# Attention pairs written out instead of looped, with weight loads and the handover to the feed-forward part in another order

## What is computed

```python
scores = scale * np.matmul(q, k.transpose(0, 1, 3, 2))      # 4 x 8 x 576 x 576
scores = np.where(block_i >= block_j, scores, -1e9)
attn = softmax(scores); x = attn @ v                         # -> 2304 x 512
gate = sigmoid(x @ w_gate); x = (gate * (x @ w_val)) @ w_out # d_ff 1536
e = argmax(x @ moe2_w_gate); out = p_e * relu(x @ w1[e]) @ w2[e]
```

## Time and profile before

| | us |
|---|---|
| median of 3 runs | 920.15 (918.3 to 922.79) |
| the profiled execution, its own time | 919.3 |
| its span, first to last instruction | 917.6 |
| attention part, up to the first feed-forward product | 196.35 |
| from there to the end of the span | 721.2 |

### The profile page before, as it was taken

One profiled execution on the slowest core, in us unless ns is written; L12 is line 12 of the kernel. 1 busy time (PEld: TensorE's weight loads), 2 busy tenths in 40 slices (PEclk: granted clock), 3 DMA queues, 4 the chain that ended last, 5 costly groups with the idle time before them and its releaser, 6 DMA issues.

```text
span 917.6 us, 15686 instructions
## 1 busy us (share of the span) xinstructions
PE 883.9 (96%) x5202; PEld 731.4 (80%) x5203; DVE 465.3 (51%) x1084; ACT 299.8 (33%) x694; POOL 215.9 (24%) x233
## 2 busy tenths in 40 slices
PE   7989998999999999999999999999999999999995
PEld 3545454569999999999999999999878888888884
DVE  5767775752124335334433543575484536483252
ACT  4545554543222113112112111223333424362141
POOL 4133335322112111211211211122112222221221
PEclk9999999999999999999999999999999999999998
DMA  4544455532412002002000100024336446474110
GB/s 138 166 125 162 152 162 169 165 109 77 147 46 69 1 1 69 1 1 70 1 1 20 51 1 1 35 67 143 124 132 224 138 131 194 132 242 135 46 46 29
DMA packets 48111, 85.37 MB, mean 93 GB/s; under 512 B 9255, under 2 KB 21543, under 8 KB 47920
## 3 DMA queue, kind: packets, MB, share of 16 engines
q1 hardware_dynamic: 42288, 69.34, 23.3%
q0 software_dynamic: 3360, 10.50, 3.7%
q10 hardware_dynamic: 2400, 4.72, 1.4%
HBM read 70.28 MB, written 14.78 MB: 93 GB/s over the span
## 4 chain that ended last, share of the span: by engine, by line
PE 84%; DMA 5%; DVE 4%; issue 4%; ACT 1%; POOLq 0%; SPq 0%; POOL 0%; DVEq 0%; ACTq 0%
PE bank L1467 23%; PE bank L1469 23%; PE bank L1468 23%; PE bank L1439 4%; PE bank L1400 4%; PE bank L1412 4%; DMA rinv_scratch<-rinv 2%; PE bank L1618 2%; DMA rwide<-rinv_scratch 1%; PE bank L1581 1%; DVE nmax L1020 1%; ACT prob L828 1%; DMA yg<-y_scratch,gcol 1%; DMA out<-orow,scol 1%; DVE xo L999 0%
## 5 line engine op out<-in xcount | busy, mean ns | idle before, releaser
L1467 PE MATMUL bank<-xh,w1h 128*128 128x384 f32 x576 | 193.9, 337 | 0.0
L1469 PE MATMUL bank<-xh,w1l 128*128 128x384 f32 x576 | 193.2, 335 | 0.0
L1468 PE MATMUL bank<-xl,w1h 128*128 128x384 f32 x576 | 192.9, 335 | 0.0
L727 POOL TENSOR_TENSOR hl<-hraw,hh 128x384 fp32r<-128x384 f32 x72 | 83.2, 1156 | 369.1 <-ACT hh L857 369.1
L1209 DVE TENSOR_TENSOR hraw<-hraw,bank 128x384 f32<-128x384 f32 x72 | 39.9, 554 | 238.1 <-ACT hraw L902 237.8
L902 ACT ACTIVATE hraw<-bank 128x384 f32<-128x384 f32 x72 | 35.4, 492 | 236.9 <-PE bank L1469 236.9
L1467 PEld LDWEIGHTS bank<-xh,w1h 128*128 128x128 f32 x576 | 108.2, 188 | 2.4
L1468 PEld LDWEIGHTS bank<-xl,w1h 128*128 128x128 f32 x576 | 108.2, 188 | 2.2
L1469 PEld LDWEIGHTS bank<-xh,w1l 128*128 128x128 f32 x576 | 108.1, 188 | 0.0
L828 ACT ACTIVATE prob<-bank,nmax 128x576 f32<-128x576 f32 (+2 forms) x144 | 75.9, 528 | 88.3 <-DVE nmax L1020 85.4
L1469 PE MATMUL bank<-woh,hl 128*128 128x512 f32 x216 | 85.4, 395 | 0.0
(11 more groups left out here) (201 smaller groups left out, 1348.1 us busy)
## 6 DMA issues: line engine op xcount, KB each, us to landing
stage<-in_we SPq DMA_DIRECT2D x56, 512.0 KB, 4.2
w1raw<-in_w SPq DMA_DIRECT2D x8, 768.0 KB, 4.5
kt<-in_kT SPq DMA_DIRECT2D x16, 288.0 KB, 3.3
qt<-in_qT SPq DMA_DIRECT2D x16, 288.0 KB, 3.8
rwide<-rinv_scratch SPq DMA_DIRECT2D x32, 144.0 KB, 2.9
xt_scratch<-xo SPq DMA_DIRECT2D x16, 288.0 KB, 2.2
xraw<-xt_scratch SPq DMA_DIRECT2D x6, 768.0 KB, 4.5
y_scratch<-yrow ACTq DMA_DIRECT2D x6, 768.0 KB, 5.1
```

Of the source, the lines that this page charges most:

```text
L727: pool.tensor_tensor(hl[:, f % 2, :], hraw[:, f % 2, :], hh[:, f % 2, :].bitcast(F32), ALU.subtract).then_inc(h_low, 1)
L1467: pe.matmul(out_, wh, ah, start=first, stop=False, skip_group_check=True)
L1468: pe.matmul(out_, wh, al, start=False, stop=False, skip_group_check=True)
L1469: return pe.matmul(out_, wl, ah, start=False, stop=last, skip_group_check=True)
```

## The change

On all engines pairs 4 to 11 are written out like the others, so no loop, and no number that is worked out in a register, is left in the attention part. `apart` is no longer called on TensorE, nor in the attention part by SyncE and GpSimd.

- **Weights.** `w1raw` number k is issued in SyncE's turn of pair 2k + 2 instead of 2k + 1, right behind `rwide` and ahead of V; number 7 in the turn of pair 15. `wr_sb` moves from behind pair 3 to just ahead of `xraw` and pair 12.
- **Start.** ScalarE issues the first Q; SyncE issues the first K, then K and Q of pair 1, then V of both.
- **ScalarE.** The copy of block 4 is made after the exponential of block 8 instead of block 7.
- **Handover.** `up(0, 0)` goes ahead of the turns of blocks 5 and 6, `up(0, 1)` is cut in two halves around the turns of blocks 7 and 8, and `pv` comes last. The first two pieces of `w_out` are loaded early, into tiles that are free then (`yT` and the last row block of `yrow`). ScalarE's last copy and VectorE's last `o_out` move behind the first sigmoid and the second gate product.

The diff, without the lines that repeat the written-out loop on the other engines:

```diff
@@ -357,7 +357,7 @@
         OUT_V = {0: (1, 5), 1: (1, 7), 3: (0, 0), 4: (0, 1), 5: (0, 2), 6: (0, 3)}
-        OUT_A = {0: (1, 6), 2: (1, 8), 3: (0, 0), 7: (0, 4)}
+        OUT_A = {0: (1, 6), 2: (1, 8), 3: (0, 0), 8: (0, 4)}
         W1_STEP = 4
@@ -379,6 +379,11 @@
+        def wo_raw(f):
+            if f < 2:
+                return [yT[:].rearrange("p c n -> p (c n)"), yrow[:, GM - 1, :]][f]
+            return woraw[:, f % 2, :]
@@ -508,55 +513,64 @@
                 sp.wait_ge(rinv_done, g + 1)
-                apart(sp)
                 sp.dma_start(rinv_dram[par].rearrange("h q i -> (h q) i"), rinv[:, par, 0:NB]).then_inc(rinv_stored, 16)
...
                 sp.wait_ge(rinv_stored, 16 * (g + 1))
-                apart(sp)
-                if not (isinstance(g, int) and g == 0):
+                if g:
                     sp.wait_ge(xo_done, g)
-                    apart(sp)
                 for h in range(2):
...
+            def w1_load(k):
+                if k:
+                    sp.wait_ge(w1_low, k)
+                sp.dma_start(w1raw[:], w1[k:k + 1].rearrange("a p f -> p (a f)")).then_inc(w1_loaded, 16)
...
                     sp.wait_ge(scores_done, NB * (g - 1))
+                    qk_load(g, p)
+                    rinv_store(g - 2, p % 2)
+                    rwide_load(g - 2, p % 2)
+                    if p % 2 == 0:
+                        w1_load(g // 2 - 1)
+                    elif g == NPAIR - 1:
+                        w1_load(2 * C - 1)
+                    sp.wait_ge(pv_done, g - 1)
+                    v_load(g, p)
+                if p >= 2:
+                    o_store(b, p - 2)
+                elif b:
+                    o_store(b - 1, p + 2)
+            def qk_load(g, p):
                 sp.dma_start(kt[p % 2][:], qkv_at(kT, g)).then_inc(qk_loaded[p % 2], 16)
                 sp.dma_start(qt[p % 2][:], qkv_at(qT, g)).then_inc(qk_loaded[p % 2], 16)
-                if not early:
-                    rinv_store(g - 2, p % 2)
-                    rwide_load(g - 2, p % 2)
-                    sp.wait_ge(pv_done, g - 1)
+            def v_load(g, p):
                 sp.dma_start(vt[p % 2][:, 0:KT_N - 1, :],
...
                              ).then_inc(v_loaded[p % 2], 16)
-                if p >= 2:
-                    o_store(b, p - 2)
-                elif not (isinstance(b, int) and b == 0):
-                    o_store(b - 1, p + 2)
-                if p % 2 == 1:
-                    k = 2 * b + p // 2
-                    if not (isinstance(k, int) and k == 0):
-                        sp.wait_ge(w1_low, k)
-                    sp.dma_start(w1raw[:], w1[bass.ds(k, 1)].rearrange("a p f -> p (a f)")).then_inc(w1_loaded, 16)
-            for p in range(PPB):
-                pair(0, p)
-            sp.dma_start(wr_sb[:], wr.rearrange("(c p) e -> p c e", p=P)).then_inc(wr_loaded, 16)
-            with sp.Fori(1, BATCH - 1) as b:
+            sp.dma_start(kt[0][:], qkv_at(kT, 0)).then_inc(qk_loaded[0], 16)
+            qk_load(1, 1)
+            v_load(0, 0)
+            v_load(1, 1)
+            for b in range(BATCH - 1):
                 for p in range(PPB):
                     pair(b, p)
+            sp.dma_start(wr_sb[:], wr.rearrange("(c p) e -> p c e", p=P)).then_inc(wr_loaded, 16)
@@ -572,18 +586,22 @@
+            def wo_load(k):
+                sp.dma_start(wo_raw(k), w_out[k * P:(k + 1) * P, :]).then_inc(wo_loaded[k % 2], 16)
+            wo_load(0)
+            wo_load(1)
             o_store(BATCH - 1, PPB - 2)
...
             sp.wait_ge(pv_done, NPAIR)
-            sp.wait_ge(scores_done, NB * NPAIR)
-            for k in range(FC):
-                if k == 2:
+            for k in range(2, FC):
+                if k == 4:
                     o_store(BATCH - 1, PPB - 1)
-                if k >= 2:
-                    sp.wait_ge(wo_high, k - 1)
-                    sp.wait_ge(wo_low, k - 1)
-                sp.dma_start(woraw[:, k % 2, :], w_out[k * P:(k + 1) * P, :]).then_inc(wo_loaded[k % 2], 16)
+                sp.wait_ge(wo_high, k - 1)
+                sp.wait_ge(wo_low, k - 1)
+                wo_load(k)
                 if k == FC // 2:
@@ -700,7 +718,6 @@
                     pool.wait_ge(qk_loaded[p % 2], 16 * (g - p % 2) + 32)
-                    apart(pool)
                     pool.tensor_scalar(kt[p % 2][:], kt[p % 2][:], SCALE, None, ALU.mult).then_inc(kt_scaled, 1)
@@ -806,6 +821,8 @@
         def _(act):
+            act.dma_start(qt[0][:], qkv_at(qT, 0)).then_inc(qk_loaded[0], 16)
@@ -832,9 +849,7 @@
-            for p in range(PPB):
-                pair(0, p)
-            with act.Fori(1, BATCH - 1) as b:
+            for b in range(BATCH - 1):
                 for p in range(PPB):
@@ -846,7 +861,6 @@
             after_unit(NPAIR - 1, 1, 6)
-            after_unit(NPAIR - 1, 1, 8)
             act.wait_ge(scores_done, NB * NPAIR)
@@ -900,9 +914,11 @@
                     act.activation(hraw[:, f % 2, :], gv_psum(f)[0], ACT.Sigmoid).then_inc(sig_done, 1)
+                    if first and f == 0:
+                        after_unit(NPAIR - 1, 1, 8)
                     if first:
                         act.wait_ge(wo_loaded[f % 2], 16 * (f // 2 + 1))
-                        act.copy(woh[:, f, :], woraw[:, f % 2, :]).then_inc(wo_high, 1)
+                        act.copy(woh[:, f, :], wo_raw(f)).then_inc(wo_high, 1)
                     if not first and f == route_steps(G)[2]:
@@ -1207,11 +1221,11 @@
                     dve.tensor_tensor(hraw[:, f % 2, :], hraw[:, f % 2, :], val_ps, ALU.mult).then_inc(hraw_done, 1)
-                    if first and f == 0:
+                    if first and f == 1:
                         o_out(NPAIR - 1, 1)
                         dve.wait_ge(wo_high, f + 1)
-                        dve.tensor_tensor(wol[:, f, :], woraw[:, f % 2, :], woh[:, f, :].bitcast(F32),
+                        dve.tensor_tensor(wol[:, f, :], wo_raw(f), woh[:, f, :].bitcast(F32),
                                           ALU.subtract).then_inc(wo_low, 1)
@@ -1389,7 +1403,6 @@
                     pe.wait_ge(exp_done, NB * (g - 1) + 7 + 2 * k)
-                apart(pe)
                 for j in SUPER[k]:
@@ -1468,7 +1478,7 @@
-            def up(G, f):
+            def up(G, f, ms=(0, 1)):
@@ -1476,14 +1486,15 @@
                     pe.wait_ge(hraw_done, n - 1)
-                for m in range(2):
+                for m in ms:
                     for c in range(C):
...
                                      xh[:, c, :], xl[:, c, :], c == 0, c == C - 1)
-                last.then_inc(gv_done, 1)
+                if ms[-1] == 1:
+                    last.then_inc(gv_done, 1)
@@ -1646,15 +1657,16 @@
+            pe.wait_ge(exp_done, NB * NPAIR - 2)
+            up(0, 0)
             turn(NPAIR - 1, PPB - 1, NB - 4)
             turn(NPAIR - 1, PPB - 1, NB - 3)
-            pe.wait_ge(exp_done, NB * NPAIR - 2)
-            up(0, 0)
+            pe.wait_ge(exp_done, NB * NPAIR)
+            up(0, 1, [0])
             turn(NPAIR - 1, PPB - 1, NB - 2)
             turn(NPAIR - 1, PPB - 1, NB - 1)
+            up(0, 1, [1])
             pv(NPAIR - 1, PPB - 1, list(range(KT_N)))
-            pe.wait_ge(exp_done, NB * NPAIR)
-            up(0, 1)
             for G in range(NG):
             pe.wait_ge(yg_high, 1)
```

More of the change, by code:

```diff
@@ L293, in bass_attention_ffn_moe @@
         gcol_done = sem("gcol_done")
-        pool_steps, pe_steps, sp_steps = sem("pool_steps"), sem("pe_steps"), sem("sp_steps")
+        pool_steps, sp_steps = sem("pool_steps"), sem("sp_steps")
         cols_done = sem("cols_done")
@@ L480, in apart @@
         def apart(eng):
-            eng.sem_inc({id(nc.gpsimd): pool_steps, id(nc.tensor): pe_steps, id(nc.sync): sp_steps}[id(eng)], 1)
+            eng.sem_inc({id(nc.gpsimd): pool_steps, id(nc.sync): sp_steps}[id(eng)], 1)
         ROUTE_OPS, SLOT_OPS, SPREAD_OPS, GATE_OPS, FIRST_OPS, ROWS_OPS = 7, 8, 2 * GM, 6, 17, 5
@@ L711, in pair @@
                     x_split()
-            for p in range(PPB):
-                pair(0, p)
-            with pool.Fori(1, BATCH - 1) as b:
+            for b in range(BATCH - 1):
                 for p in range(PPB):
@@ L1028, in pair @@
                         o_out(g - 1, (p - 1) % 2)
-            for p in range(PPB):
-                pair(0, p)
-            with dve.Fori(1, BATCH - 1) as b:
+            for b in range(BATCH - 1):
                 for p in range(PPB):
@@ L1456, in pair @@
                         pv(g - 1, p - 1, PV_STEP[i])
-            for p in range(PPB):
-                pair(0, p)
-            with pe.Fori(1, BATCH - 1) as b:
+            for b in range(BATCH - 1):
                 for p in range(PPB):
```

## The result

| | before | after |
|---|---|---|
| median of 20 runs, us | 920.11 (916.41 to 923.77) | 911.63 (906.27 to 918.31) |
| profiled execution, its span | 919.3, 917.6 | 914.98, 913.1 |
| attention and handover, up to `up(0, 2)` | 208.84 | 203.38 |

The account below looks back on a forecast made before the run. TensorE, busy 96% of the span, was taken as the bound, with only idle time and half clock to win. Gains 9.0 + 2.1 + 0.3 + 1.55 = 12.95 us off 919.3 gave 906.35, rounded up to 906.5; range 901.5 to 911.5.

Parts of the forecast that it names:

- Weights moved: Attention pairs: weight loads no longer ahead of rinv stores, so pairs 4, 6, 8, 10, 14 become calm; 9.0 us gained.
- Rival 3: Attention pairs: the weights' new place disturbs as much as the old one, rwide slowed; 912 us, chance 0.08.
- `xraw`, 3.77: Pair 12: xraw and wr_sb still stand ahead of rinv, so pair 4's loss of 3.77 us is left there.
- rival 1: Pair 12: stall shorter than 1.8 us, no half clock, 3.77 becomes 1.47; 904.1 us, chance 0.20.
- Semaphore steps, 2.1: Attention pairs: loop written out and semaphore steps gone, 0.14 us a pair over 15 pairs, 2.1 us gained.
- Rival 2: Attention pairs: only the transfer order moves, nothing gained for semaphores; 908.5 us, chance 0.10.
- rival 5: Attention pairs: TensorE's waits count more, 0.36 us a pair, and the clock holds at pair 12; 900.8 us, chance 0.08.
- The copy: Attention pairs: ScalarE's copy behind the last exponential removes TensorE's 0.29 us wait, but VectorE's chain is next; nothing counted.
- Start: Kernel start: Q issued by ScalarE need not stand behind K's issue; 0.3 us gained, bounds 0.43 gained, 0.3 lost.
- Handover: End of attention: TensorE's waits of 0.37, 0.65 and 0.56 us go; 1.55 us gained, bounds 1.0 and 2.0.
- Behind the handover, 0: Everything behind the handover: TensorE's order is the same and nothing it waits for comes later, so taken as fixed.
- Rival 4: Attention, odd pairs: GpSimd becomes the gate, K scaled 1.8 us too late, half clock too; 930 us, chance 0.04.

Follow-up runs that it names:

- e8: Changed kernel without VectorE's 1e-9 addition, the eight weight loads back at their old places on SyncE's queue: 914.52 us, ratio 0.9933 to the kernel before.
- e10: Kernel before with only the six weight loads moved and without the 1e-9 addition: 910.36 us, ratio 0.9883.
- e1: Changed kernel without VectorE's 9-element addition of 1e-9 to the row sums: 903.54 us, ratio 0.983 to the kernel before.
- e5: Changed kernel without the 1e-9 addition, TensorE's semaphore steps put back: 906.62 us, ratio 0.9843 to the kernel before.
- e7: Changed kernel without the 1e-9 addition, old handover order back, early w_out loads kept: 908.33 us, ratio 0.9859 to the kernel before.
- e18: Changed kernel, GpSimd's splits 0 to 6 wait for the addition, xraw and wr_sb issued in pair 13's turn: 903.76 us, ratio 0.981.
- e17: Changed kernel, splits wait for the next pair's first row maximum, row sums after the fourth, a maximum replacing the addition: 916.83 us, ratio 0.9951.
- e6: Changed kernel without the 1e-9 addition, ScalarE's copy of block 4 back ahead of the last exponential: 905.11 us, ratio 0.9843.
- e4: Changed kernel with the 1e-9 addition replaced by a maximum over one element: 908.56 us, one run.
- e11: Changed kernel without the 1e-9 addition, the start as before: 906.98 us, ratio 0.9835 to the kernel before.
- e12: Changed kernel with the addition, GpSimd's splits 0 to 6 waiting for the next pair's first row maximum: 907.14 us, ratio 0.9836.
- e14: Changed kernel, row-sum block one row maximum later, the addition replaced by a maximum over one element: 908.32 us, ratio 0.9857.
- e15: Changed kernel, splits 0 to 6 wait for the next pair's first row maximum, xraw and wr_sb issued in pair 13's turn: 905.61 us, ratio 0.9836.

## Why the prediction was wrong

- **Weights moved, 9.0: the step that failed is the one on their cover.** "Spare: about 3 us. This is the cover that makes the move free" priced GpSimd's 4.9 us only for what waits for GpSimd. It didn't ask what runs beside it on VectorE now. The move is worth what I said or more (9.5 to 11.0 in e8, 10.4 in e10) and 8 us come back through the addition (911.63 against 903.54). Weights that were split by the addition's time are now split at it, 0.5 us ahead of the mark by my own estimate and 0.2 behind it in the profile (27.61 against 27.38); the rows of the addition and of `w1l` in the trace of before would have shown a margin of 0.03 us. For K, which the cover was priced for, it held: K of pair 3 was scaled 7.0 us behind the mark, where I had 6.1 and a need at 9.3.
- **Rival 3 gave the right time, 912, for the wrong cause.** It had `rwide` slowed by the weights behind it; even pairs 4, 6, 8 and 14 are calm, and e1, with the same queue, has no such loss.
- **`xraw`, 3.77: right** (4.1 in pairs 11 and 12 of the profile). Whether the clock falls there changes between executions: rival 1's outcome in e1, not in after.
- **Semaphore steps, 2.1: sound, undersized.** 2.7 us, 0.18 a pair. I costed the one step on the chain and left those between turns at 0.06; how the 0.18 divides between them no run shows. Rival 2 (nothing) falls by e5, and rival 5 by its 0.36 us a pair. The copy is worth 0, as said.
- **Start, 0.3: not to be told from 0.** Q is issued earlier and lands later; that fits K of pair 1 sharing the transfer engines, the risk I named, but no run shows it apart.
- **Handover, 1.55: undersized.** The three waits in the earlier trace rows add to 1.58. 2.1 were won between the two profiles, and 2.5 by e7, of which its three waits are 1.9.
- **Behind the handover, 0: not quite.** From `up(0, 2)` to the end of the span 708.8 us became 709.7, with a half clock that the part did not have before (see the last section); in e1, without it, it was 707.8.
- **Rival 4**, K late, falls: even e18, with the split of pair 2 starting 2.2 us later than in the changed kernel, doesn't wait.

With the collisions out, the sum would have been 919.3 less 9.0, 2.7 and 2.5: 905.1 where e1 has 903.5.

## What to carry to other kernels

Before moving a long GpSimd instruction, list what VectorE does in the new stretch and in the old: a small `tensor_scalar` on the path can be held for the whole of it, and a margin of 0.03 us in the old place is luck, not design. Two delays with one cause can protect each other, so removing the cause can make a new meeting. A wait that orders the two (e18) won back about 6 of the 8 us (7.9 less the 1.9 of `xraw`), with 1.3 us between the highest and the lowest of its four runs; what it left was a meeting with a cast that no wait orders.

## What the hardware showed that I had not expected

- An addition over 9 elements a partition took 3.19 us beside a subtraction of 3.43. Row maxima and copies out of `bank` kept their 0.4 to 0.7 us beside such subtractions, and the reciprocals of the same nine numbers their 0.18 (e17, from 80.30 on).
- The clock doesn't follow the length of a stall alone: 2.11 us (e1) and 1.95 (e6) left it whole, 1.30 halved it (e4), 1.81 did in the kernel before.
- The clock can fall with no pause of TensorE's ahead of it. In the routing part of the changed kernel 24 products of 8 columns run from 652.54 to 655.29, and products of 512 columns behind them are at half clock:

```profile
655.60:659.00 3.40, 3.40 (x10) 2.66 (x9) 2.35 (x13) 0.82 (x2) 0.00 (x0) 0.50 0.00 0
```

It stood in the profiles of e5, e7, e10, e11, e12, e14, e15 and e18 too, and not in those of the kernel before and the other ten. With the new handover and no half clock at it, the stretch from pair 15's first exponential to the end of the span took 729.8 to 730.8 us with it and 728.2 to 729.4 without. What sets it off stays open.
